# A float32r feed-forward kernel on one Trainium2 core: the narrow products of two tiles placed side by side on the halves of the array, in batches of four tiles

## The reference

```python
out = einsum('bshk,bskhg->bshg', softmax(weight_gen), windows_of_7(x))   # B,S,D = 2,4096,192; 8 heads
x = out.reshape(8192, 192)
xn = x / sqrt(mean(x * x) + 1e-6) * rms_g
x = (silu(xn @ w_gate) * (xn @ w_val)) @ w_out        # d_ff = 1536
h = x @ w_in                                          # d_ff = 2048
out = (h * sigmoid(1.702 * h)) @ w_out2               # [8192, 192]
```

## Time and profile before

| | |
|---|---|
| median of 3 runs | 1329.49 us (1329.16 to 1329.7) |
| span of the profiled execution | 1328.2 us, 1.3 us under the median |
| PE busy | 1283.0 us, 97% of the span |
| DVE, ACT, POOL busy | 59%, 51%, 8% |
| chain that ended last | PE 92% |

### The profile page before, as it was taken

One profiled execution on the slowest core, in us unless ns is written; L12 is line 12 of the kernel. 1 busy time (PEld: TensorE's weight loads), 2 busy tenths in 40 slices (PEclk: granted clock), 3 DMA queues, 4 the chain that ended last, 5 costly groups with the idle time before them and its releaser, 6 DMA issues.

```text
span 1328.2 us, 19585 instructions
## 1 busy us (share of the span) xinstructions
PE 1283.0 (97%) x6304; PEld 1088.3 (82%) x6304; DVE 782.2 (59%) x1186; ACT 679.0 (51%) x1194; POOL 101.7 (8%) x104
## 2 busy tenths in 40 slices
PE   0889999999999999999999999999999999999998
PEld 0667888889888888888889888888888889888898
DVE  5889475473846638475473846638475473843432
ACT  2343646555464553646555454553645555464454
POOL 6873000000000000000000000000000000000000
PEclk9999999999999999999999999999999999999999
DMA  5331000000100001000000100001000000000000
GB/s 141 87 108 39 1 16 31 16 31 4 41 0 15 30 3 41 0 15 30 15 30 3 41 0 15 30 3 41 0 15 30 15 30 0 12 0 13 1 13 13
DMA packets 14525, 32.21 MB, mean 24 GB/s; under 512 B 1828, under 2 KB 7842, under 8 KB 14496
## 3 DMA queue, kind: packets, MB, share of 16 engines
q1 hardware_dynamic: 14496, 31.85, 7.6%
HBM read 25.55 MB, written 6.29 MB: 24 GB/s over the span
## 4 chain that ended last, share of the span: by engine, by line
PE 92%; DVE 1%; issue 1%; ACT 0%; DVEq 0%
PE acc L754 15%; PE up_ps L706 11%; PE up_ps L713 11%; PE up_ps L714 11%; PE up_ps L707 11%; PE up_ps L710 11%; PE acc L755 7%; PE acc L734 3%; PE acc L731 3%; PE acc L735 3%; PE acc L732 3%; PE acc L733 3%; PE acc L768 0%; DVE hidden L654 0%; PE acc L772 0%
## 5 line engine op out<-in xcount | busy, mean ns | idle before, releaser
L669 DVE TENSOR_TENSOR h_lo<-hidden,h_hi 128x512 fp32r<-128x512 f32 x448 | 315.7, 706 | 382.0 <-ACT h_hi L487 381.5
L487 ACT CAST h_hi<-hidden 128x512 fp32r<-128x512 f32 x448 | 278.7, 622 | 186.1 <-DVE hidden L654 178.5
L754 PE MATMUL acc<-out_w,h_hi 128*128 128x384 f32 x1024 | 306.4, 355 | 0.0
L755 PE MATMUL acc<-out_w,h_lo 128*128 128x192 f32 x1024 | 257.6, 252 | 0.0
L471 ACT ACTIVATE hidden<-up_ps 128x512 f32<-128x512 f32 x256 | 153.2, 598 | 203.2 <-PE up_ps L714 202.9
L466 ACT ACTIVATE silu<-up_ps 128x512 f32<-128x512 f32 x192 | 114.5, 596 | 196.1 <-PE up_ps L714 195.7
L654 DVE TENSOR_TENSOR hidden<-silu,up_ps 128x512 f32<-128x512 f32 x192 | 131.8, 687 | 129.0 <-ACT silu L466 128.8
L755 PEld LDWEIGHTS acc<-out_w,h_lo 128*128 128x128 f32 x1024 | 195.0, 190 | 10.2
L754 PEld LDWEIGHTS acc<-out_w,h_hi 128*128 128x128 f32 x1024 | 192.2, 188 | 10.6
L706 PE MATMUL up_ps<-x_hi,up_w 128*128 128x512 f32 x384 | 154.5, 402 | 3.1 <-DVE hidden L654 2.0
L713 PE MATMUL up_ps<-x_rest,up_w 128*128 128x512 f32 x384 | 152.7, 398 | 3.8 <-DVE x_rest L593 3.8
(11 more groups left out here) (80 smaller groups left out, 1671.1 us busy)
## 6 DMA issues: line engine op xcount, KB each, us to landing
x_win<-in_x_dram SPq DMA_DIRECT2D x14, 960.0 KB
out_dram<-out_sb SPq DMA_DIRECT2D x15, 384.0 KB, 2.3
stage<-in_moe_w_out_dram SPq DMA_DIRECT2D x13, 192.0 KB, 2.5
logits<-in_weight_gen_dram SPq DMA_DIRECT2D x16, 112.0 KB, 2.0
stage<-in_moe_w_in_dram SPq DMA_DIRECT2D x4, 256.0 KB, 2.9
stage<-in_moe_w_in_dram SPq DMA_DIRECT2D x8, 128.0 KB, 2.9
stage<-in_moe_w_val_dram SPq DMA_DIRECT2D x3, 256.0 KB, 4.2
stage<-in_moe_w_val_dram SPq DMA_DIRECT2D x6, 128.0 KB, 2.8
```

The source lines that it names most:

```text
L487: nc.scalar.copy(h_hi[:, u % 4, :], hidden[:, u % 2, :]).then_inc(hi_ready, 1)
L669: nc.vector.tensor_tensor(h_lo[:, u % 4, :], hidden[:, u % 2, :], h_hi[:, u % 4, :].bitcast(F32), ALU.subtract).then_inc(lo_ready, 1)
L754: nc.tensor.matmul(acc[:, j, 0:2 * D], h_hi[:, n % 4, tile], w, start=n == 0, stop=False)
L755: ins = nc.tensor.matmul(acc[:, j, 0:D], h_lo[:, n % 4, tile], w[:, 0:D], start=False, stop=n == U2 - 1)
```

## The change

The product of the low weight part of the rest with the low part of x is dropped; with it the lo product of the rest has only 64 rows (weight lo on x hi). The low rest weights of two tiles are stored one above the other in `pair_lo` (partitions 0 to 63 and 64 to 127), and a second copy of the rest of x hi is made on partitions 64 to 127 (`x_twin`, `y_twin`). So the two tiles' 64-row products use the upper and the lower half of the array. PE no longer goes unit by unit: it makes the four whole-array matmuls of each of four tiles (two gated units, or four of the second layer), then the four half-array ones, then the down products of the units of the batch before. `up_done` is counted on the half-array products. The lists of steps on DVE and ACT stay as they are, but for one copy of 64x512 in each `split_rest`, and each split of weights on POOL waits for the split before it.

```diff
-        up_w = sb("up_w", [P, 2 * U1 + U2, 4, P], F32R)
+        up_w = sb("up_w", [P, 2 * U1 + U2, 3, P], F32R)
+        pair_lo = sb("pair_lo", [P, PAIRS, P], F32R)
+        x_twin, y_twin = sb("x_twin", [P, N], F32R), sb("y_twin", [P, N], F32R)
...
                 nc.vector.tensor_copy(rest[0:REST, :], f32[0:REST, 1, :]).then_inc(hi_sem, 1)
+
+                nc.vector.tensor_copy(twin[REST:P, :], f32[0:REST, 1, :])
...
+                if n:
+                    pool.wait_ge(chunk_split, n)
...
                 nc.tensor.matmul(ps[:, :], w[:, 2, :], rest[:, :], start=False, stop=False)
-                return nc.tensor.matmul(ps[:, :], w[:, 3, :], rest[:, :], start=False, stop=True)
+
+            def up_halves(ps_a, ps_b, pair, rest, twin):
+
+                a = nc.tensor.matmul(ps_a[:, :], pair_lo[0:REST, pair, :], rest[0:REST, :], start=False, stop=True)
+                b = nc.tensor.matmul(ps_b[:, :], pair_lo[REST:P, pair, :], twin[REST:P, :], start=False, stop=True)
+                return a, b
...
+                for u in (u for u in slots if u < U1 and u % 2 == 0):
+                    if is_block(i, 0):
+                        pe.wait_ge(chunk_split, chunks_for_up(u, True))
+                    for v in (u, u + 1):
+                        if v >= 2:
+
+                            pe.wait_ge(silu_done, i * U1 + v - 1)
+                            pe.wait_ge(prod_done, i * U1 + v - 1)
...
+                            up_full(gate, v, x_hi, x_lo, x_rest)
+                        up_full(val, U1 + v, x_hi, x_lo, x_rest)
+                    for v in (u, u + 1):
+                        gate, val = up_ps[2 * (v % 2):2 * (v % 2) + 2]
+                        _, last = up_halves(gate, val, v, x_rest, x_twin)
+                        last.then_inc(up_done, 1)
+
+                    if u == 0 and not (is_block(i, 0) or is_block(i, 1)):
+
+                        for n in range(U2 - 4, U2):
+                            down2(i - 1, n)
+                    if mixing and u == U1 - 2:
+                        turn_x(i + 1)
+                    if u:
+                        down1(i, u - 2)
+                        down1(i, u - 1)
+
+                for n in range(0, U2, 4) if UNITS - 1 in slots else ():
+                    if is_block(i, 1):
+                        pe.wait_ge(chunk_split, chunks_for_up(n, False))
+                    for m in (n, n + 2):
+                        if n or is_block(i, GROUPS):
+
+                            pe.wait_ge(gelu_done, i * U2 + (m - 2 - U2))
...
+                    for m in (n, n + 2):
+                        even, odd = up_halves(up_ps[m % 4], up_ps[m % 4 + 1], U1 + m // 2, y_rest, y_twin)
+                        even.then_inc(up_done, 1)
+                        odd.then_inc(up_done, 1)
+                    if n == 0 and slots[0] == 0:
+                        down1(i, U1 - 2)
+                        down1(i, U1 - 1)
+                    if n:
+                        for m in range(n - 4, n):
+                            down2(i, m)
```

More of the change, by code:

```diff
@@ L51, in mix_and_two_ffns @@
     UNITS = U1 + U2
+    PAIRS = U1 + U2 // 2
     BATCH_P = S // OWN
@@ L121, in staged_count, with even_splits @@
         return sum(32 if chunks[q][1] == "rest" else 16 for q in range(c + 1) if place_of(q) == place_of(c))
+    def even_splits(n):
+        return sum(chunks[q][0] is w_in and chunks[q][1] == "rest" for q in range(n + 1))
     def chunks_for_up(m, gated):
@@ L351, in split_chunk @@
                 parts = split_parts(src, kind, t)
+                if n:
+                    pool.wait_ge(chunk_split, n)
                 if hi_here:
                     pool.wait_ge(staged[place_of(n)], staged_count(n))
-                    for hi, _, f in parts:
-                        last = nc.gpsimd.tensor_copy(hi, f)
+                    for hi, f, _, _, _ in parts:
+                        if hi is not None:
+                            last = nc.gpsimd.tensor_copy(hi, f)
                     last.then_inc(chunk_hi, 1)
                 pool.wait_ge(chunk_hi, n + 1)
-                for hi, lo, f in parts:
+                for a, (_, _, lo, f, hi) in enumerate(parts):
+                    if a and kind == "rest":
+                        pool.wait_ge(even_split, even_splits(n))
                     last = nc.gpsimd.tensor_tensor(lo, f, hi.bitcast(F32), ALU.subtract)
+                    if a == 0 and kind == "rest" and len(parts) > 1:
+                        last.then_inc(even_split, 1)
                 last.then_inc(chunk_split, 1)
@@ L383, in _ @@
                 split_chunk(n, False)
+            pool.wait_ge(chunk_split, RMS0_AT)
             rms(0)
@@ L399, in chunk_hi_half @@
                 act.wait_ge(staged[place_of(n)], staged_count(n))
-                for hi, _, f in split_parts(places[place_of(n)], kind, t):
-                    last = nc.scalar.copy(hi, f)
+                for hi, f, _, _, _ in split_parts(places[place_of(n)], kind, t):
+                    if hi is not None:
+                        last = nc.scalar.copy(hi, f)
                 last.then_inc(chunk_hi, 1)
@@ L699, in _, with up_full @@
         def _(pe):
-            def up(ps, t, hi, lo, rest, hi_sem=None, ready=None, g=None):
+            def up_full(ps, t, hi, lo, rest, hi_sem=None, ready=None, g=None):
                 w = up_w[:, t, :, :]
@@ L789, in run @@
                         elif is_block(i, 1):
-                            pe.wait_ge(silu_done, U1 - 1 + u)
-                            pe.wait_ge(prod_done, U1 - 1 + u)
+                            pe.wait_ge(silu_done, U1 - 1 + v)
+                            pe.wait_ge(prod_done, U1 - 1 + v)
                         elif not is_block(i, 0):
-                            pe.wait_ge(gelu_done, i * U2 - (U2 + 2 if u == 0 else U2))
-                        pair = up_ps[2 * (u % 2):2 * (u % 2) + 2]
@@ L819, in run @@
-                    if u == 0 and not (is_block(i, 0) or is_block(i, 1)):
-                        down2(i - 1, U2 - 3)
-                        down2(i - 1, U2 - 2)
-                    if u == 1 and not (is_block(i, 0) or is_block(i, 1)):
-                        down2(i - 1, U2 - 1)
-                    if mixing and u == X_T:
-                        turn_x(i + 1)
-                    if slots[0] == 0 and 2 <= u < U1 + 2:
-                        down1(i, u - 2)
-                    if u >= U1 + 3:
-                        down2(i, u - U1 - 3)
+                            pe.wait_ge(gelu_done, i * U2 - (U2 + 2 if v == 0 else U2))
@@ L840, in _ @@
             for tiles in (range(0, 2), range(2, 4)):
-                for n in range(U2 - 3, U2):
+                for n in range(U2 - 4, U2):
                     down2(GROUPS, n, tiles)
```

71 lines of the change are left out of this document (36 added, 35 removed).

## The result

The changed kernel takes 1410.35 us (median of 4 runs, 1409.15 to 1413.16) against 1329.6 us: the ratio is 1.0604, 95% interval 1.0589 to 1.0619. The profiled execution has a span of 1409.2 us, 81.0 more than before, and 1410.98 us in all. The forecast was 1385 us and slower. It is slower, by 81 us instead of 55: inside the range of 1342 to 1422, but outside the 1362 to 1402 of the likeliest case.

The account below looks back on a forecast made before the run. PE's program was taken as the bound. A middle block summed -4.70 + 3.20 + 0.81 + 2.14 + 1.38 + 0.24 = +3.07, +40 over 13; with the other blocks +55 on 1328.2, so 1385 us, range 1342 to 1422.

Parts of the forecast that it names:

- the likeliest case: Switches near 0.16 us each plus the forecast waits, 1362 to 1402 us; chance 0.45.
- What is removed: On PE, two half-array products side by side replace two whole-array matmuls per pair of tiles: -4.70 us per block.
- Switches: On PE, 20 changes per block between whole and half array, 0.16 us each: +3.20 us per block.
- a): Gated batch to gated batch: PE's wait for the odd unit's banks, nothing at a switch of 0.16 us.
- b): At u = 8, behind the squares: PE waits 0.81 us for prod(9), once a block.
- c): At u = 10: PE's transposes, directly behind the half products, wait 2.14 us for DVE's scaling.
- d): At n = 4 of the second layer: PE waits 1.38 us for GELU(3), ACT being held by down product 11.
- The lower clock: Rival: behind the stop before the transposes, ten matmuls per block run at 1.2 GHz, 26 us more, 1411; chance 0.05.
- the stop at 59.80: A shorter PE stop in the kernel before; the next matmul was 0.31 us on, not 0.43, cited against a clock fall.
- dear switches (0.28): Rival: each switch costs emptying and weight load, 0.28 us, giving 1419; chance 0.18 shared with halves in turn.
- halves in turn: Rival: a pair's halves run one after the other, 75 us more, 1420; chance 0.18 shared with dear switches (0.28).
- The rival on the other side: Faster: switches free and the transposes' wait hidden, 1315; the whole saving without any wait would be 1254; chance 0.10.

Follow-up runs that it names:

- e4_same: Changed kernel with both half-array products of a pair on the upper half of the array, so they can't run at once; 1471.15 us in one run.
- e8_split: e7_all with each pair's half-array products directly behind its own whole-array matmuls, four switches per batch of four tiles instead of two; 1380.57 us in one run.
- e11_whole_moved: e9_evac2 with whole-array products in place of the half-array ones; 1342.65 us in one run.
- e1_turn: Changed kernel with the transposes of the mix behind the down products of units 8 and 9 instead of ahead of them; 1363.73 us.
- e2_fill: Changed kernel with six extra whole-array matmuls on PE ahead of its wait for the scaling, except before the first three transposes; 1393.1 us.
- e9_evac2: e7_all, but DVE empties its part of the accumulator at u = 14, ahead of split_x, while ACT's copy stays at u = 15; 1334.43 us.
- e7_all: Changed kernel with transposes behind down products of units 8 and 9, accumulator emptied at u = 15, squares behind silu(9); 1353.06 us.
- e6_square: Changed kernel with ACT's four squares between silu(9) and h_hi(9) instead of between h_hi(8) and silu(9); 1392.81 us in one run.

## Why the prediction was right, and where it was short

- What bounds the kernel: right. PE's program sets the time, and its waits are where the forecast had them.
- What is removed: right, 0.235 per pair, side by side; e4_same shows it. The Trainium skill, page "TensorE: Matmul & The Clock Gate", Part 3, says that matmuls on different row groups run together. The trace agrees: the starts are 0.01 us apart.
- Switches: the kind was right, the size short. 0.16 was taken, the emptying alone; the trace has 0.195, whole blocks give 0.19 to 0.20 (e8_split, e11_whole_moved). For 20 switches that is 0.7 us per block more. The Trainium skill, page "TensorEngine Tiling (Array Packing)", Key Properties, says that a change of mode drains TensorE. The trace is in accord with this: the distance grows on both sides of each change, by 0.09 and 0.105.
- Waits, start to start and less 0.235: a) some 0.03 at each odd unit (none forecast); b) 556.72 to 557.73 in the changed kernel, 0.78 (forecast 0.81); c) 560.12 to 562.70, 2.15 behind the switch (2.14); d) 575.89 to 577.31, 1.19 (1.38: ACT's step from h_hi(1) to GELU(2) was 0.52 and not 0.63, and PE went on 0.65 and not 0.74 behind the GELU).
- The step that failed: the sum had no term for the clock. The lower clock was set up as a rival in place of the forecast, with a chance of 0.05 and 26 us. It came on top of the forecast. The argument against it (no slow matmul behind the stop at 59.80) used a stop of 1.2 us for one of 2.2. e1_turn and e2_fill show that it hangs on the stop. 14 such stretches at 85.1 - 83.5 = 1.6 us are 22 of the 26 us that the sum fell short.
- Luck: the rival's 1411 is next to the 1410 measured, but it had ten slow matmuls in 13 blocks for the eight behind 14 transposes, and the dearer switches made up the difference. And the time lies in the band of 1402 to 1430, given to dear switches (0.28) or halves in turn, of which neither happened.
- The balance of the spans: blocks 0 and 1 are 7.5 us longer from transposes to transposes (13 had been estimated), the next 13 periods 67.6 (40), what follows 6.5 (about 2; one slow stretch is in it), and the first transposes come 0.6 earlier: 81.0. Of the 27.6 that the 13 periods are over, 12 with the lower clock give 18.7. The rest is 0.7 per block: 0.7 for the switches and 0.1 at odd units, less 0.2 by which b) and d) were shorter; 0.1 is not accounted for.
- The rival on the other side, a kernel that gains because nothing waits: e9_evac2 removes the three long waits and the clock's fall in the middle blocks, and gains 0.35 us a block. By the forecast's own terms it would have been 79.77 - 4.70 + 3.20 = 78.27, 1.5 less than before; the dearer switches (0.7) and the short waits that are left (0.3) took most of it. The last 0.1 us was not followed up; e11_whole_moved has it too (80.04 against 79.77, of which 0.2 are its short waits).

## What to carry to other kernels

When one engine is the bound and others hand buffers back to it, a batch that hands them on together has to be followed through each queue: here 4.7 us of saved matmuls a block met 3.9 us of switches and 4 us of waits, and it took moves on three queues (PE's transposes, ACT's squares, the emptying of the accumulator on ACT and DVE) to bring the waits down to 0.3. Weigh products on half the array against the two switches they cost: with four half products between switches the gain was 0.47 us less 0.39. A span in which an engine shows as busy throughout can still hold short waits: distances between starts show them. And a stop of the bounding engine costs more than its length if the clock falls behind it.

## What the runs showed of the hardware

- Changing between whole-array and 64-row float32r matmuls costs 0.195 us each way (0.19 to 0.20 by whole blocks), in two parts, ahead of the first matmul and behind it; two 64-row matmuls on the two halves start 0.01 us apart and cost 0.235 together.
- Behind a stop of 2.2 us PE ran at the lower of its two levels for some eight matmuls (0.43 us apart), beginning 0 to 1.4 us after it had gone on; behind the stop of 0.5 us in e2_fill and those of 1.3 us in e7_all (14 of them) it did not. The stop was of nearly one length in all middle blocks, but not every one had the slow stretch: 14 of 15 in the changed kernel, every second one in e6_square.
- Six useless matmuls per block in a stop of PE made this kernel 17 us faster (e2_fill, 1410.35 to 1393.1 us).
